# Last stage of a long-convolution and gated-MLP kernel: side work placed behind g and Exp, the transposes of x*y behind the projection

## The reference

```python
# x, v: (2, 12480, 128); pos_emb: (12480, 64)
h_mlp  = np.maximum(pos_emb @ w1, 0.0) @ w2
h_filt = h_mlp * np.exp(-0.01 * pos)[:, None]
u = x * v
y = irfft(rfft(u, 2S) * rfft(h_filt, 2S))[:, :S]      # causal convolution along the sequence
t = (x * y).reshape(24960, 128)
h = t @ w_in                                          # 128 -> 2048
P = a[0] + a[1]*h + a[2]*h**2 + a[3]*h**3
Q = 1.0 + |b[0]|*|h| + |b[1]|*h**2
out = (P / (Q + 1e-06)) @ w_out                       # 2048 -> 128
```

## Time and profile before

| | |
|---|---|
| median of 3 runs | 2199.3 us |
| the profiled execution | 2197.26 us |
| its span in the trace | 2195.5 us |
| busy PE / DVE / ACT / POOL | 2032.1 / 1803.5 / 1822.5 / 1894.3 us |
| L637 POOL den x480 | 946.3 us busy, 1971 ns each |
| L629 POOL slope x480 | 500.8 us busy, 1043 ns each |
| L797 DVE g x480 | 516.3 us busy, 1076 ns each |
| L764 DVE num x480 | 518.0 us busy, 1079 ns each |

### The profile page before, as it was taken

How to read it: one execution, slowest core, us unless ns; L and a number is a source line. 1 busy time by engine, 2 the same in 40 slices (tenths; PEclk the granted TensorE clock), 3 DMA queues, 4 the chain that set the end, 5 groups by cost and what they waited for, 6 DMA issues and landing times. The chain is left out here.

```text
span 2195.5 us, 33367 instructions
## 1 busy us (share of the span) xinstructions
PE 2032.1 (93%) x8964; PEld 1456.4 (66%) x8964; DVE 1803.5 (82%) x2271; ACT 1822.5 (83%) x2431; POOL 1894.3 (86%) x1218
## 2 busy tenths in 40 slices
PE   7999499999969999999999999999999999999997
PEld 4777499999946666666666666666666666666664
DVE  4888488888748888888888888888888888888887
ACT  4888466666549999999999999999999989999997
POOL 3777388888749999999999999999999999999997
PEclk9999799999969999999999999999999999999999
DMA  6999766666531111111111111111111111111100
GB/s 181 308 302 309 189 162 174 175 175 174 130 79 31 31 31 30 30 30 30 30 30 30 34 30 30 30 35 46 35 30 30 30 30 30 30 30 30 30 9 15
DMA packets 65730, 175.10 MB, mean 80 GB/s; under 512 B 5046, under 2 KB 8414, under 8 KB 62686
## 3 DMA queue, kind: packets, MB, share of 16 engines
q1 hardware_dynamic: 65694, 174.67, 29.2%
HBM read 102.89 MB, written 71.76 MB: 80 GB/s over the span
## 5 line engine op out<-in xcount | busy, mean ns | idle before, releaser
L637 POOL TENSOR_TENSOR den<-slope,mag 128x832 f32<-128x832 f32 x480 | 946.3, 1971 | 43.5 <-POOL slope L629 6.9
L890 PE MATMUL acc_p<-g_s,w_out_k 128*128 128x416 f32 x1920 | 784.2, 531 | 88.6 <-DVE g_s L797 83.8
L764 DVE SCALAR_TENSOR_TENSOR num<-square,level,h_p 128x832 f32<-128x832 f32 x480 | 518.0, 1079 | 89.6 <-ACT square L671 78.4
L629 POOL TENSOR_SCALAR slope<-mag,den_c 128x832 f32<-128x832 f32 x480 | 500.8, 1043 | 98.1 <-ACT mag L662 69.7
L797 DVE SCALAR_TENSOR_TENSOR g_s<-num,ratio,r_p 128x832 f32<-128x832 f32 x480 | 516.3, 1076 | 83.3 <-ACT r_p L688 54.9
L890 PEld LDWEIGHTS acc_p<-g_s,w_out_k 128*128 128x128 f32 x1920 | 332.6, 189 | 373.8 <-issue 221.9
L671 ACT ACTIVATE square<-h_p,centre 128x832 f32<-128x832 f32 x480 | 459.2, 957 | 128.5 <-DVE mag L759 112.2
L879 PE MATMUL h_p<-xy_hi,w_lo 128*128 128x416 f32 x960 | 459.2, 478 | 5.2 <-DVE num L764 4.0
L681 ACT ACTIVATE den<-den 128x832 f32<-128x832 f32 x480 | 431.0, 898 | 0.0
L688 ACT ACTIVATE r_p<-den 128x832 f32<-128x832 f32 x480 | 417.5, 870 | 12.9 <-DVE g_s L797 12.9
L879 PE MATMUL h_p<-xy_lo,w_hi 128*128 128x416 f32 x960 | 338.2, 352 | 0.0
(11 more groups left out here) (79 smaller groups left out, 2807.2 us busy)
## 6 DMA issues: line engine op xcount, KB each, us to landing
bent<-bent_s SPq DMA_DIRECT2D x60, 576.0 KB, 6.1
bin_s<-bent SPq DMA_DIRECT2D x24, 1440.0 KB, 9.8
x_s<-in_x SPq DMA_DIRECT2D x60, 416.0 KB
back<-back_s SPq DMA_DIRECT2D x24, 960.0 KB, 7.9
vin_s<-back SPq DMA_DIRECT2D x30, 768.0 KB, 6.0
v_s<-in_v SPq DMA_DIRECT2D x30, 416.0 KB
out<-o_s SPq DMA_DIRECT2D x60, 208.0 KB
pos_s<-in_pos_emb SPq DMA_DIRECT2D x30, 88.0 KB
```

The costliest lines, as they stand in the source:

```text
L629: nc.gpsimd.tensor_scalar(slope[:, q % DEEP], mag[:, q % DEEP], den_c[:, 1:2], den_c[:, 0:1], ALU.mult, ALU.add).then_inc(slope_done, 1)
L637: nc.gpsimd.tensor_tensor(den[:, q % DEEP], slope[:, q % DEEP], mag[:, q % DEEP], ALU.mult).then_inc(den_done, 1)
L764: nc.vector.scalar_tensor_tensor(out=num[:, q % NUMS], in0=square[:, q % SQUARES], scalar=level[:], in1=h_p[:, q % 2, :, 0:TOK], op0=ALU.a ...
L890: mm = nc.tensor.matmul(acc_p[:, 0:TOK], w_out_k[:, ft], g_s[:, q % DEEP, t], start=(ft == 0), stop=(ft == FT - 1))
```

## The change

Five things are moved; no instruction is added or taken away, and the arithmetic is the same.

- In ACT's step, the o copy and `split_hi` stand before `from_h` (directly behind Exp) in place of behind it.
- In DVE's step, |h| and g come first, then `sums`, `times_x` and `split_lo`, then num.
- `turn_in` on PE stands between `project` and `hidden` in place of behind `hidden`.
- `times_x` and `turn_in` of the first half move from step 3 to step 4.
- The second half's `rows` moves from step 6 to 5, and its `split_hi` and `split_lo` from step 9 to 8.

```diff
-            UNFOLD, TIMES_X, TURN_IN, SPLIT_HI, SPLIT_LO = (2, 6), (3, 7), (3, 7), (5, 9), (5, 9)
+            UNFOLD, TIMES_X, TURN_IN, SPLIT_HI, SPLIT_LO = (2, 5), (4, 7), (4, 7), (5, 8), (5, 8)
             SUMS, TURN_OUT, LEAVE = (0, 8), (0, 12), (2, 14)
...
                     reciprocal(i, q)
-                    if ahead:
-                        from_h(i + (q + LEAD_E) // PER, (q + LEAD_E) % PER)
                     if m in LEAVE:
...
                     if more and m in SPLIT_HI:
                         half = SPLIT_HI.index(m)
                         split_hi((blk + 1) * 2 + half, (q // BLOCK_PAIRS + 1) % SLOTS, half)
+                    if ahead:
+                        from_h(i + (q + LEAD_E) // PER, (q + LEAD_E) % PER)
...
+                    if ahead and (q + LEAD_E) % 2:
+                        magnitude(i + (q + LEAD_E) // PER, (q + LEAD_E) % PER)
+                    activation(i, q)
                     if m in SUMS:
                         c = blk * BATCH + SUMS.index(m) - 1
                         if positive(c + 1):
                             sums(c)
-                    if ahead and (q + LEAD_E) % 2:
-                        magnitude(i + (q + LEAD_E) // PER, (q + LEAD_E) % PER)
-                    activation(i, q)
...
+                    if more and m in TIMES_X:
+                        times_x(nxt + TIMES_X.index(m), i + (q // BLOCK_PAIRS + 1) // SLOTS, s, TIMES_X.index(m))
+                    if more and m in SPLIT_LO:
+                        split_lo(nxt + SPLIT_LO.index(m), s, SPLIT_LO.index(m))
                     if ahead:
                         numerator(i + (q + LEAD_E) // PER, (q + LEAD_E) % PER)
-                        side()
-                    else:
-                        side()
...
                     project(i, q)
+                    nxt, s = (blk + 1) * 2, (q // BLOCK_PAIRS + 1) % SLOTS
+                    if more and m in TURN_IN:
+                        turn_in(nxt + TURN_IN.index(m))
                     if ahead:
                         hidden(i + (q + LEAD_H) // PER, (q + LEAD_H) % PER)
...
-                    if more and m in TURN_IN:
-                        turn_in(nxt + TURN_IN.index(m))
```

More of the change, by code:

```diff
@@ L903, in step @@
                     project(i, q)
+                    nxt, s = (blk + 1) * 2, (q // BLOCK_PAIRS + 1) % SLOTS
+                    if more and m in TURN_IN:
+                        turn_in(nxt + TURN_IN.index(m))
                     if ahead:
                         hidden(i + (q + LEAD_H) // PER, (q + LEAD_H) % PER)
-                    nxt, s = (blk + 1) * 2, (q // BLOCK_PAIRS + 1) % SLOTS
                     if more and m in UNFOLD:
```

## The result

| | before | after |
|---|---|---|
| median | 2199.1 us (4 runs, 2197.7 to 2200.1) | 2226.0 us (4 runs, 2225.7 to 2226.4) |
| span of the profiled execution | 2195.5 us | 2223.8 us |
| after / before | | 1.0123, 95% interval 1.0105 to 1.0140 |

What follows compares the result with a forecast made beforehand. Bound: a cycle through ACT and DVE, 6.22 us per two steps. Adding 2.95 and removing 2.10 gave +0.85 us a block, +25 over 29 blocks: 2197.3 to 2222, plus 2 for the median, 2224 us; range 2193 to 2241.

Steps and rivals of the forecast that it cites:

- The cycle: Chain of waits through ACT and DVE closing every two steps, 6.22 us; only work put on it costs, at full length.
- What the change takes away: Delays in steps 8 and 9, 0 and 5 from side work on DVE and ACT disappear: -2.10 us a block.
- The term for step 0: Part of the removed time: `oT` on DVE, in front of g, no longer delays step 0, 0.36 us a block.
- DVE, nothing: Side work moved on DVE fits its rooms or is covered by ACT's lateness in step 8, so it adds nothing.
- The o copies, +0.48 twice: On ACT, copies between Exp and |h| of steps 2 and 14 find no room: 0.96 us a block added.
- The waits: ACT's `split_hi` waits for PE's transposes in steps 5 and 8, adding 0.69 and 1.30 us a block.
- E: The start of `square` on ACT in an even step, from which the prediction counts its times.
- The rule on matmul spacing: N/2.4 + 2.5 ns per matmul: four transposes in 0.18 us, each wait 0.34 shorter, some 20 us less; not used.
- Rival 1: Transposes are ready in time and ACT never waits, so the kernel is faster, 2178 us; chance 0.12.
- rival 2: PE on time but not early: first wait vanishes, second is 0.63; -0.11 us a block, 2196 us; chance 0.08.
- Rival 3: PE falls further behind as DVE's side work precedes num; waits grow by 0.3 each, 2241 us; chance 0.14.
- Rival 4: The o copies on ACT are hidden after all, waits as forecast: -0.96 us a block, 2196 us; chance 0.02.

Runs made afterwards that it cites:

- the first experiment: The changed kernel with only the o copies (steps 2 and 14) moved back behind `from_h`; 2198.1 us, ratio 1.0004 to the kernel before.

## Why the prediction was right

The forecast was 2224 us, the result 2226.0, with a block 0.97 us longer where 0.85 was reckoned. The mechanism is the one forecast, with small errors in two terms. That the total is only 2 us off is in part luck: the profiled execution was put at 2222 and took 2225.7, and the median was put 2 us above it and lay 0.3 above. By its steps:

- **The cycle.** 6.22 us per two steps holds in every kernel here, whatever stands beside it. It is the same in the changed kernel (6.21), with the transposes late (6.21), and where nothing costs on top of it (49.78 a block).
- **What the change takes away.** 2.10 a block. Shown as a whole by the kernel with ACT's side work put back: it has the other moves, pays 0.50 again in step 5, and its block is 1.5 us shorter than before the change where 1.6 is left of the 2.10. The term for step 0 was too large. Of its 0.36, 0.11 belonged to the sums (what the kernel with the sums in front loses over the changed one), 0.1 didn't go away (below), and the rest, some 0.15 by difference, was the o copy of step 14.
- **DVE, nothing.** Nearly so. In step 8 DVE even waits 0.72 behind `oT` and `xy_lo`. But the room of 0.59 in even steps, read from step 14, is 0.1 smaller in steps 0, 4 and 12: `xy` of step 4 overran it by 0.12, not by the 0.02 that was left out, and cost nothing only because `split_hi` waited behind it. With that cover gone it cost 0.10.
- **The o copies, +0.48 twice.** Measured 0.47 and 0.48, and 28 us when they were moved back (0.96 x 29 is 28).
- **The waits.** `project` of step 4 was put 1.37 after E and came at 1.40 (1290.03 - 1287.88 - 0.75); `split_hi` at 3.33 and came at 3.35; cost 0.69, measured 0.71. In the second half `project` of step 7 was put at 4.41 and came at 4.44 (1299.99 - 1294.80 - 0.75), `split_hi` at 6.37 and came at 6.39; cost 1.30, measured 1.35. That the 1.40 for transposes behind a queued projection was derived from one row and a difference of lengths was the weakest step, and it held: 1.39 and 1.40.
- **The rule on matmul spacing.** By the section "Back-to-back issue gap" of the Trainium skill's "TensorE: Matmul & The Clock Gate" four transposes were estimated at 0.18 us. The same section gives the formula for an isolated matmul and says that it counts too little at small N, where weight loads take time as well. The comparison was also uneven: 0.18 is the spacing of four starts, while the 0.52 of the row runs from the first start to the last end. In the changed kernel four transposes last 0.52 again and hold PE for 0.30 (1291.42 to 1291.72). The waits are those of the row, so the rule gave no ground for waits 0.34 shorter.
- **What was missing.** Step 0 was to cost nothing, and costs 0.09 in one block of two (6.79 here, 6.70 in the next). It does so in the kernel before too (6.58 and 6.51), so it was wrongly counted among what goes away. In part it is the smaller room on DVE: num starts 1.03 and 1.02 after E in the two blocks, not 0.99. The rest, only in the long block, is the step from DVE's |h| to ACT's `square`, which starts 0.11 after the end of |h| in place of 0.03. Why it does so every second time isn't shown. It is worth 1.3 us over 29 blocks.

Rival 1 (no waits) and rival 2 (PE on time) fall with the 0.85 us before `split_hi`. Rival 3 (PE further behind) falls with the projections' starts, 0.03 off. Rival 4 falls with the first experiment. The spread of 2215 to 2233 given for the forecast was a little narrow for its own reason: 0.1 us on each of four terms is up to 0.4 a block, 12 us to each side.

## What to carry to other kernels

When several engines are all over 80% busy and none is full, look for the chain that closes on itself across them: write down the starts of one period from the timelines and find where each instruction starts just as another ends. In these kernels only what was put on that chain cost time, and then all of it; the same 0.48 us copy cost nothing in an odd step and 13 us in an even one. A room read from one period can be 0.1 us smaller in the next, so read several. Before moving side work, list the rooms between the links, check that the work is ready at that point (a copy placed early but fed late blocks everything queued behind it), and check what the moved work pushes back on the engine that feeds the chain.

## What the runs showed of the hardware that was not expected

Nothing of weight. In most of the rows read here a start on ACT, DVE or PE follows the end of what it waits for by 0.03 to 0.13 us. It is longer for g behind Exp in steps 0, 4 and 12 (0.19 in place of 0.09), for DVE's `xy` behind `rows` (0.21 in the kernel before) and for POOL's slope behind ACT's |h| (0.20). The hand-overs that the prediction added up were regular enough for both starts of `split_hi` to come within 0.02 us of the reckoning.
